# q and k loaded already turned, their rounded stacks written in place by ACT and POOL, an exponential bias from the minimum, an eighth weight slot

## The chip, the cores and the metric

One core of a Trainium2 chip runs the whole program. The metric is the device time of one execution in microseconds (us). The engines are PE (matrix multiplies), DVE (vector), ACT (activations), POOL (general) and SP (here it only issues transfers). PSUM is the memory that PE writes; it has eight banks of 128 x 512 floats.

## The reference

Three stages follow each other: attention in 2 x 8 heads of 768 tokens and 64 columns, masked by a six-bit hash, then a soft mixture of eight experts, then a gated two-layer network.

```python
q_bits = (q @ proj > 0); k_bits = (k @ proj > 0)      # 6 bits each
mask = q_bucket[:, :, :, None] == k_bucket[:, :, None, :]
scores = np.where(mask, scale * q @ k.T, -1e9)
attn = np.exp(scores - scores.max(-1)); attn /= attn.sum(-1) + 1e-9
x = attn @ v                                          # to 1536 x 512
logits = x @ phi; d = softmax(logits, 0); slot_input = d.T @ x
slot_out[e] = relu(slot_input[e] @ w1[e]) @ w2[e]     # 8 experts, 4 slots each
x = softmax(logits, 1) @ slot_out
h = x @ w_in; out = (h * sigmoid(1.702 * h)) @ w_out
```

A row of the mask can be empty; its attention is then the mean of v.

## The kernel before

**Attention.** The outer loop runs over 16 heads m (head 0, a hardware loop of six rounds with two heads each, and three heads written out). Each head has six steps p, one for each tile of 128 queries. Every engine has its own written order. In step p, PE waits until the exponentials of tile p are there, multiplies the scores of the tile two further on (`target`: p+2, or tile 0 or 1 of the next head) at line 653, and turns the probabilities of tile p with six transposes at line 663. In steps 0 and 1 it also multiplies the previous head's turned probabilities with v (line 673), in step 0 the hashes of the next head (line 637), in step 2 it turns the previous head's output back (line 683). DVE finds the maximum of a row of scores (line 1046) and makes a bias of it (line 1049); ACT takes the exponential with that bias (line 933) and copies turned probabilities out of PSUM (line 927); DVE copies some of them (line 1040). There are two buffers of scores and two of probabilities, so an engine can run about one step ahead of the next.

**Stacks.** The scores are a sum of products of rounded ("high") and remainder ("low") parts. For each head four stacks of 128 x 768 hold them: `stack_a1` (q high twice), `stack_b1` (k high, k low), `stack_a2` (q low, hash bits), `stack_b2` (k high, hash bits). The four are there twice, for even and odd heads. Before, q and k of head m+2 come in with tokens on the partitions; PE turns them in step 4 (line 629), ACT and DVE copy them out (lines 946 and 1057), POOL makes `high` and `low` (lines 560 and 567), and SP places them in the stacks with six transfers (lines 442 and 448). DVE compares the hashes (line 1075) and SP places the bits with four transfers (line 433).

**Empty rows.** The sum of v over all tokens (POOL line 575, PE line 645, DVE line 1083) times a factor for empty rows (DVE line 1097) is added to the output by POOL (lines 585 and 591).

**Experts and the last network.** Weights come as 20 numbered fills, mostly of 2 MB. There are 11 slots for them, seven in `ring_lo` and four in memory that attention leaves free. Fills 0 to 5 are loaded inside the loop. A fill from 11 on has to wait until an expert has used up the slot (`REUSE`). Line 816 is the first product of an expert, line 835 the second, line 878 the first product of the last network, lines 892 to 914 the rest. PE also runs matmuls on `ones` that nobody reads (line 622), in places where it would stand idle.

Of the kernel before, what the change touches and what calls it, by code (L numbers as in the profile page):

```python
# [23 lines left out]
F32 = mybir.dt.float32  # L24
# [5 lines left out]
P = 128  # L30
BANK = 512
BIG = 2.0 ** 40
MASKED = -8e9
# [3 lines left out]
def kernel_program(nc, q, k, v, proj, phi, w1, w2, w_in, w_out, out):  # L37
    B, H, S, D = q.shape
    NB = proj.shape[1]
# [21 lines left out]
    assert D * 2 == P and TILES % 2 == 0 and SL == QUAD and CH == NQ and 3 * NB <= QUAD and HD == BANK and G * BANK == N  # L61

    bh = lambda x: x.rearrange("b h s d -> (b h) s d")
    q_dram, k_dram, v_dram = bh(q), bh(k), bh(v)

    with ExitStack() as ctx:
# [8 lines left out]
        LO = 7  # L75
        FOUR = 4
        PLACES = TILES + 2
        ARENA = (3 + 2 * FOUR + 2) * S + 2 * TILES * D + HC + TILES * PLACES * P
# [6 lines left out]
        ident = sb("ident", [P, P])  # L85
        stack_i = sb("stack_i", [P, SL])
        ones = sb("ones", [P, P])
        proj_w = sb("proj_w", [P, 2 * QUAD])
        small_at = -(-nc.sbuf_base // 32) * 32
        small = sb("small", [P, HC])  # L90
        hash_c = sb("hash_c", [P, 2])
        max_raw = sb("max_raw", [P, 2, TILES])
        neg_max = sb("neg_max", [P, 2, TILES])
        row_sum = sb("row_sum", [P, 2, TILES])
        empty = sb("empty", [P, TILES])
        denom = sb("denom", [P, TILES])
        recip = sb("recip", [P, TILES])
        e_recip = sb("e_recip", [P, TILES])
        v_part = sb("v_part", [P, 2, D])
        v_sum = sb("v_sum", [P, 2, D])  # L100
# [14 lines left out]
        high = rounded("high", arena_at, [P, S])  # L115
        uniform = arena[:, 0:HC].rearrange("p (t d) -> p t d", t=TILES)
        at[0] = S
        nat = part(S).rearrange("p (t f) -> p t f", t=TILES)
        low = rounded("low", arena_at + 4 * at[0], [P, S])
        qk = part(S)  # L120
# [5 lines left out]
        PROBS_AT = at[0]  # L126
# [5 lines left out]
        low_first = rounded("low_first", arena_at + 4 * PROBS_AT, [P, S])  # L132
        nat_second = probs[:, 1, :].rearrange("p (t f) -> p t f", t=TILES)
# [3 lines left out]
        SLOTS = 11  # L137
        PLACE = (0, 3, 1, 4, 2, 5, 6, 7, 8, 9, 10)
        A_AT = HC
# [10 lines left out]
        REUSE = (0, 2, 4, 1, 6, 3, 8, 5, 7)  # L150
# [25 lines left out]

        slot_t = v_part[:, :, :].rearrange("p r d -> p (r d)").rearrange("p (c s) -> p c s", c=CH)
        out_t = v_sum[:, :, :].rearrange("p r d -> p (r d)").rearrange("p (c s) -> p c s", c=CH)

        hid_t = x_flat[:, SLOT + N:SLOT + N + 2 * HK * SL].rearrange("p (w k s) -> p w k s", w=2, k=HK)  # L180


# [1087 lines left out]
```

## Time and profile before

| | |
|---|---|
| median of 3 runs | 479.94 us (479.64 to 482.36) |
| the profiled execution | 482.05 us, of which the span of the trace is 480.3 us |
| PE busy | 460.0 us (96%) |
| DVE busy | 304.0 us (63%) |
| ACT busy | 226.8 us (47%) |
| POOL busy | 108.7 us (23%) |
| moved by the transfers | 76.76 MB |

The trace lists instructions with their start and duration. A row of the timeline merges repeats (x4), says in brackets how long the engine sat idle before it and which engine released it. Roughly, attention lasts to 262 us of the span, logits and slot sums to 282, the experts to 325, the last network to the end.

### The profile page before, as it was taken

What the parts mean: (1) busy time and instruction counts of PE and PEld (TensorE: products, weight loads), DVE (VectorE), ACT (ScalarE), POOL (GpSimd) and SP (SyncE); (2) the same over time, 40 slices, a digit from 0 to 9 for tenths busy, and PEclk for the clock granted to TensorE, in tenths of its full rate; (3) what the DMA queues carried; (4) which work ended last, traced back from release to release, by engine and by line L of the source; (5) the groups of instructions that cost most, each with busy time, mean ns of one, the idle gap of its engine ahead of it and who ended that gap; (6) DMA issues with size and microseconds to landing.
All of it is one profiled execution on the core that took longest, in us unless ns stands there. A gap on an engine that the chain in (4) does not pass through costs nothing.

```text
span 480.3 us, 8550 instructions
## 1 busy us (share of the span) xinstructions
PE 460.0 (96%) x2939; PEld 341.5 (71%) x2939; DVE 304.0 (63%) x582; ACT 226.8 (47%) x476; POOL 108.7 (23%) x194
## 2 busy tenths in 40 slices
PE   7789999999999999999999999689999999999997
PEld 6577678776687766777675754236788888888885
DVE  3377778777787777877763440105999486648661
ACT  1376667866678666786664331115633221121110
POOL 4234344443444434444311000000000000000000
PEclk9799999999999999999999999999999999999999
DMA  5547768767776677773685659997000110010002
GB/s 139 142 114 206 185 190 234 193 206 197 197 213 196 202 192 203 214 199 106 195 294 186 253 202 373 396 409 285 1 0 2 44 45 0 2 72 16 1 0 87
DMA packets 55833, 76.76 MB, mean 160 GB/s; under 512 B 29313, under 2 KB 33281, under 8 KB 55297
## 3 DMA queue, kind: packets, MB, share of 16 engines
q1 hardware_dynamic: 55808, 76.44, 51.4%
q8 instruction: 15, 0.25, 0.2%
q14 instruction: 10, 0.07, 0.1%
HBM read 51.45 MB, written 3.15 MB: 114 GB/s over the span
## 4 chain that ended last, share of the span: by engine, by line
PE 88%; DMA 7%; DVE 2%; SPq 1%; ACT 1%; issue 1%; ACTq 0%; DVEq 0%
PE ps L653 16%; PE ps L673 13%; PE ps L663 12%; PE ps L912 9%; PE ps L914 9%; PE ps L913 9%; DMA ring_lo<-in_moe_w 4%; PE ps L637 3%; PE ps L629 2%; PE ps L892 2%; PE ps L816 2%; PE ps L622 2%; PE ps L835 2%; PE ps L742 1%; PE ps L683 1%; DMA arena<-in_k 1%
## 5 line engine op out<-in xcount | busy, mean ns | idle before, releaser
L1046 DVE TENSOR_REDUCE max_raw<-ps 128x1 f32<-128x768 f32 x96 | 91.9, 957 | 49.5 <-PE ps L653 48.5
L653 PE MATMUL ps<-stack_b,stack_a 96*128 96x384 f32 (+1 forms) x384 | 93.5, 366 | 4.7 <-ACT arena L933 1.6
L933 ACT ACTIVATE arena<-ps,neg_max 128x768 f32<-128x768 f32 x96 | 86.8, 904 | 17.4 <-DVE neg_max L1049 16.0
L927 ACT COPY arena<-ps 128x384 f32<-128x384 f32 x144 | 64.4, 482 | 51.1 <-PE ps L663 51.0
L653 PEld LDWEIGHTS ps<-stack_b,stack_a 96*128 96x128 f32 (+1 forms) x384 | 63.5, 192 | 28.9 <-ACT arena L933 14.9
L663 PE MATMUL ps<-ident,arena 128*128 128x128 f32 x576 | 79.8, 274 | 1.1 <-ACT arena L927 1.0
L912 PE MATMUL ps<-w_high,g_high 128*128 128x512 f32 x192 | 75.0, 390 | 1.2 <-DVE g_low L1227 1.1
L914 PE MATMUL ps<-w_high,g_low 128*128 128x512 f32 x192 | 74.7, 389 | 0.0
L913 PE MATMUL ps<-w_low,g_high 128*128 128x512 f32 x192 | 74.7, 389 | 0.0
L663 PEld LDWEIGHTS ps<-ident,arena 128*128 128x128 f32 x576 | 68.9, 141 | 5.0 <-ACT arena L933 1.4
L673 PE MATMUL ps<-arena 128*64 128x384 f32 x384 | 68.0, 491 | 0.0
L1023 ACT ACTIVATE arena<-ps 128x512 f32<-128x512 f32 x48 | 28.3, 599 | 79.7 <-PE ps L892 79.7
L673 PEld LDWEIGHTS ps<-arena 128*64 128x64 f32 x384 | 25.9, 137 | 31.2 <-issue 28.7
L1237 DVE TENSOR_TENSOR arena<-ps,arena 128x512 f32<-128x512 f32 x48 | 33.0, 688 | 19.6 <-ACT arena L1023 19.5
L912 PEld LDWEIGHTS ps<-w_high,g_high 128*128 128x128 f32 x192 | 36.0, 188 | 9.7 <-issue 2.3
L914 PEld LDWEIGHTS ps<-w_high,g_low 128*128 128x128 f32 x192 | 36.0, 188 | 7.5
L913 PEld LDWEIGHTS ps<-w_low,g_high 128*128 128x128 f32 x192 | 36.0, 188 | 7.4
L567 POOL TENSOR_TENSOR low<-arena,high 128x768 fp32r<-128x768 f32 x15 | 27.3, 1818 | 35.6 <-PE ps L637 35.6
L1227 DVE TENSOR_TENSOR g_low<-arena,g_high 128x512 fp32r<-128x512 f32 x48 | 33.2, 692 | 1.7
L591 POOL TENSOR_TENSOR x_sb<-x_sb,arena 128x384 f32 (+1 forms) x16 | 16.0, 1002 | 69.1 <-DVE x_sb L1104 69.1
L1040 DVE COPY arena<-ps 128x384 f32<-128x384 f32 x48 | 26.5, 553 | 2.0 <-PE ps L663 2.0
L1225 DVE CAST g_high<-arena 128x512 fp32r<-128x512 f32 x48 | 20.5, 428 | 5.4 <-DVE arena L1237 0.9
(121 smaller groups left out, 463.6 us busy)
## 6 DMA issues: line engine op xcount, KB each, us to landing
ring_lo<-in_moe_w SPq DMA_DIRECT2D x12, 1024.0 KB, 5.5
ring_lo<-in_moe_w SPq DMA_DIRECT2D x6, 2048.0 KB, 16.7
stack_a<-high SPq DMA_DIRECT2D x32, 192.0 KB, 3.1
stack_b<-high SPq DMA_DIRECT2D x32, 192.0 KB, 3.3
arena<-in_moe_w SPq DMA_DIRECT2D x3, 2048.0 KB, 8.4
arena<-in_q SPq DMA_DIRECT2D x16, 192.0 KB, 3.2
arena<-in_k SPq DMA_DIRECT2D x16, 192.0 KB, 3.4
arena<-in_v SPq DMA_DIRECT2D x16, 192.0 KB, 2.4
```

The lines of the kernel that those rows point to most:

```text
L653: last = nc.tensor.matmul(s_ps[p % 2][:, c, :], a[r][0:used, rows], b[r][0:used, cols], start=(a is stack_a1), stop=(a is stack_a2))
L663: last = nc.tensor.transpose(ring[b][:, j * P:(j + 1) * P], probs[:, p % 2, kt * P:(kt + 1) * P], ident[:, :])
L673: last = nc.tensor.matmul(o_ps[x * D:(x + 1) * D, :], nat_v[:, r, kt, :], probs_t[:, at:at + HALF, kt, :], start=(kt == 0), stop=(kt == TI ...
L912: nc.tensor.matmul(ps[:, 4 + tt, :], g_high[:, s % DEEP, rows], w_h, start=(fi == 0), stop=False)
L913: nc.tensor.matmul(ps[:, 4 + tt, :], g_high[:, s % DEEP, rows], w_l, start=False, stop=False)
L914: last = nc.tensor.matmul(ps[:, 4 + tt, :], g_low[:, s % DEEP, rows], w_h, start=False, stop=(fi == FC - 1))
L927: nc.scalar.copy(probs_t[:, place(r, p), b * HALF:(b + 1) * HALF, :], ring[b].rearrange("p (a s) -> p a s", a=HALF)).then_inc(t_taken[b], 1)
L933: nc.scalar.activation(probs[:, p % 2, :].rearrange("p (c s) -> p c s", c=2), s_ps[p % 2], ACT.Exp, bias=neg_max[:, r, p:p + 1], scale=SCA ...
L1023: nc.scalar.activation(sig[:, s % 4, :], ps[:, fi % 4, :], ACT.Sigmoid, scale=1.702)\
L1046: nc.vector.tensor_reduce(max_raw[:, r, p:p + 1], s_ps[p % 2], axis=AX.XY, op=ALU.max)\
L1227: nc.vector.tensor_tensor(g_low[:, s % DEEP, :], gated[:, s % 2, :], g_high[:, s % DEEP, :], ALU.subtract)\
L1237: nc.vector.tensor_tensor(gated[:, s % 2, :], ps[:, fi % 4, :], sig[:, s % 4, :], ALU.mult)\
```

## The change

The host hands over q and k already turned and each twice over the 128 partitions (`qk`), and all constants in one tensor (`consts`). ACT and POOL (in head 0 DVE too) write the rounded parts straight into the stacks, with a column of `const` as scale. SP's six placing transfers, PE's transposes of q and k and the copies out of PSUM are gone. The signs and the scale of the scores are in the stacks, so that masked products are large and positive: DVE takes the minimum, makes a scale (-1, or 0 for an empty row) and a bias of it in two small instructions, and ACT's exponential has the scale and the bias as columns. A row that is empty gives exp(0) = 1 everywhere, so the sum of v and its addition are gone. The bits are scaled by POOL in place. `ring_lo` has eight slots, so there are 12. Fill 6 goes out in head 0, fills 7, 8 and 9 in the last three heads. The number of `ones` matmuls at the start changes.

```diff
-        LO = 7
+        LO = 8
...
-        SLOTS = 11
+        SLOTS = 12
...
-        REUSE = (0, 2, 4, 1, 6, 3, 8, 5, 7)
+        REUSE = (0, 2, 4, 1, 6, 3, 8, 5)
...
             def body(m, r, k):
+                if within(m, 2) and (not isinstance(m, int) or m > 0):
+                    sp.wait_ge(hash_ready, m + 2)
+                    sp.wait_ge(k_again, m + 2)
+                    load_qk(m + 2, r, both)
                 if within(m, 1):
                     place_bits(m + 1, 1 - r)
-                    place_low(m + 1, 1 - r, low)
...
-                if within(m, 3):
-                    sp.wait_ge(qk_turned[1], m + 3)
-                    load_qk(m + 3, 1 - r, nat)
-                if within(m, 2):
-                    sp.wait_ge(scores_ready, m * TILES + TILES)
-                    place_high(m + 2, r)
...
+            def low_q(n, r, src):
+
+                pool.wait_ge(q_high, n + 1)
+                nc.gpsimd.tensor_tensor(stack_a2[r][lower, :], src[lower, 0, :], stack_a1[r][lower, :], ALU.subtract)\
+                    .then_inc(q_low, 1)
...
             def body(m, r, k):
                 if within(m, 1):
-                    split_low_of(m + 1)
-                if within(m, -1):
-                    finish(m - 1, 1 - r, k + r - 1)
-                if within(m, 1):
-                    fold_v(m + 1, 1 - r, k + r)
+                    scale_bits(m + 1)
                 if within(m, 2):
-                    if not isinstance(m, int) or m > 0:
-                        pool.wait_ge(x_done, m + K0)
-                    split_high_of(m + 2, r, k + r + 1)
+                    pool.wait_ge(qk_in[r], (k + 2) * 2 * DMA)
+                    pool.wait_ge(scores_ready, m * TILES + TILES)
+                    high_k(r, both)
+                    low_q(m + 2, r, both)
+                    low_k(m + 2, r, both)
+                    nc.gpsimd.tensor_tensor(stack_b2[r][lower, :], both[lower, 1, :], over(k_scale, lower), ALU.mult)\
+                        .then_inc(k_again, 1)
...
+                for j in range(NQ):
+                    last = nc.tensor.matmul(hash_ps[j * QUAD:(j + 1) * QUAD, :], proj_w,
+                                            src[:, j % 2, (j // 2) * HC:(j // 2 + 1) * HC], start=True, stop=True)
...
-                    if p == TILES - 2 and within(m, 2):
-                        pe.wait_ge(hash_taken, m + 2)
-                        if not isinstance(m, int) or m > 0:
-                            pe.wait_ge(x_scaled, m)
-                        turn_qk(m + 2, r, k + 1, nat)
...
-                    if p == TILES - 1:
-                        sum_v(m, r)
...
-                                     bias=neg_max[:, r, p:p + 1], scale=SCALE,
+                                     bias=exp_bias[:, r, p:p + 1], scale=exp_scale[:, r, p:p + 1],
...
+            high_q_and_k_again(0, both)
+            act.wait_ge(hash_taken, 1)
+            for j in range(NQ):
+                rows = slice(j * QUAD, (j + 1) * QUAD)
+                last = nc.scalar.activation(
+                    (stack_a2, stack_b2)[j % 2][0][D:D + QUAD, (j // 2) * HC:(j // 2 + 1) * HC],
+                    bits[rows, :], ACT.Copy, scale=bit_times[rows, :])
...
-                    if p == TILES - 2 and within(m, 2):
-                        take_qk(m + 2, r, k + r + 1)
                     take_tile(m, r, p, 0)
                     if p % 2 == 0:
                         take_tile(m, r, p, 1)
                     if p + 2 < TILES or within(m, 1):
                         act.wait_ge(t_ready[1], m * TILES + p + 1)
                         exps(*target(m, r, k, p))
+                    if p == HALF and within(m, 2):
+                        act.wait_ge(qk_in[r], (k + 2) * 2 * DMA)
+                        nc.scalar.activation(stack_a1[r][:, :], both[:, 0, :], ACT.Copy, scale=q_scale).then_inc(q_high, 1)
...
-                nc.vector.tensor_reduce(max_raw[:, r, p:p + 1], s_ps[p % 2], axis=AX.XY, op=ALU.max)\
-                    .then_inc(max_found, 1)
-                dve.wait_ge(max_found, g + 1)
-                nc.vector.tensor_scalar(neg_max[:, r, p:p + 1], max_raw[:, r, p:p + 1], MASKED, -SCALE,
-                                        ALU.max, ALU.mult).then_inc(max_ready, 1)
...
+                nc.vector.tensor_reduce(low, s_ps[p % 2], axis=AX.XY, op=ALU.min).then_inc(min_found, 1)
+                dve.wait_ge(min_found, g + 1)
+                nc.vector.tensor_scalar(exp_scale[:, r, p:p + 1], low, EMPTY, -1.0, ALU.is_lt, ALU.mult)\
+                    .then_inc(scale_found, 1)
+                dve.wait_ge(scale_found, g + 1)
+                nc.vector.tensor_scalar(exp_bias[:, r, p:p + 1], low, exp_scale[:, r, p:p + 1], -1.0, ALU.mult, ALU.mult)\
+                    .then_inc(min_ready, 1)
```

Two places show what this does to the order. On ACT, in the first head of a loop round, from the exponential of step 3 to that of step 4 (L933, L842: exponential; L927, L836: turned probabilities; L946: half of q and k). Before:

```order
L927 COPY arena<-ps 128x384
L932 REGISTER_ALU
L933 ACTIVATE arena,row_sum<-ps,neg_max 128x768
L943 REGISTER_ALU
L945 ISA
L946 COPY arena<-ps 128x384
L927 COPY arena<-ps 128x384 x2
L932 ISA
L933 ACTIVATE arena,row_sum<-ps,neg_max 128x768
```

Of the change:

```order
L836 COPY arena<-ps 128x384
L841 REGISTER_ALU
L842 ACTIVATE arena,row_sum<-ps,exp_bias,exp_scale 128x768
L887 ISA
L888 ACTIVATE stack_a_50<-arena,const 128x768
L836 COPY arena<-ps 128x384 x2
L841 ISA
L842 ACTIVATE arena,row_sum<-ps,exp_bias,exp_scale 128x768
```

The copy of 384 columns ahead of step 4's two copies has given way to one of 768 columns from SBUF, in the same place between two exponentials.

On DVE, steps 2 and 3 of the same head (L1046, L969: reduction; L1104, L994: scaling of the previous head's output). Before:

```order
L1046 TENSOR_REDUCE max_raw<-ps 128x1
L1049 TENSOR_SCALAR neg_max<-max_raw 128x1
L1104 ISA
L1104 TENSOR_TENSOR x_sb<-ps,recip 128x6x64
L1045 REGISTER_ALU
L1046 TENSOR_REDUCE max_raw<-ps 128x1
L1049 TENSOR_SCALAR neg_max<-max_raw 128x1
L1040 COPY arena<-ps 128x384
```

Of the change:

```order
L969 TENSOR_REDUCE low_raw<-ps 128x1
L971 TENSOR_SCALAR exp_scale<-low_raw 128x1
L974 TENSOR_SCALAR exp_bias<-low_raw,exp_scale 128x1
L991 REGISTER_ALU
L994 ISA
L994 TENSOR_TENSOR x_sb<-ps,recip 128x6x64
L967 REGISTER_ALU
L969 TENSOR_REDUCE low_raw<-ps 128x1
L971 TENSOR_SCALAR exp_scale<-low_raw 128x1
L974 TENSOR_SCALAR exp_bias<-low_raw,exp_scale 128x1
L962 COPY arena<-ps 128x384
```

Behind every reduction stand two small instructions instead of one, the second of which reads what the first wrote.

## Rows read from the trace of the kernel before

**Rows 1.** Page, TensorE's granted clock in 40 slices, tenths of full speed.
```profile
PEclk9799999999999999999999999999999999999999
```
**Rows 2.** Timeline, one head: start us, duration us, engine, line, what, [idle before].
```profile
63.48 0.97 PE L653 MATMUL ps<-stack_b,stack_a 128*128 128x384 f32 x4
...
71.41 0.96 PE L653 MATMUL ps<-stack_b,stack_a 128*128 128x384 f32 x4
...
73.53 0.56 DVE L1104 TENSOR_TENSOR x_sb<-ps,recip 128x384 f32 x1
...
75.10 0.15 DVE L1049 TENSOR_SCALAR neg_max<-max_raw 128x1 f32<-128x1 f32 x1
...
75.29 0.90 ACT L933 ACTIVATE arena<-ps,neg_max 128x768 f32<-128x768 f32 x1 [0.33 <-DVE neg_max L1049]
...
75.45 0.82 PE L629 MATMUL ps<-ident,arena 128*128 128x128 f32 x6
...
76.11 0.82 PE L663 MATMUL ps<-ident,arena 128*128 128x128 f32 x6
76.18 0.47 ACT L946 COPY arena<-ps 128x384 f32<-128x384 f32 x1
...
77.38 0.92 ACT L933 ACTIVATE arena<-ps,neg_max 128x768 f32<-128x768 f32 x1
...
78.13 0.33 PE L645 MATMUL ps<-v_part,ones 128*128 128x64 f32 x2
...
78.44 0.97 PE L653 MATMUL ps<-stack_b,stack_a 128*128 128x384 f32 x4
```
**Rows 3.** The same timeline, small DVE instructions beside a POOL subtraction.
```profile
65.99 1.81 POOL L567 TENSOR_TENSOR low<-arena,high 128x768 fp32r<-128x768 f32 x1 [1.99 <-PE ps L637]
...
66.66 1.18 DVE L1089 TENSOR_SCALAR empty<-max_raw 128x6 f32<-128x6 f32 x1
...
67.87 0.17 DVE L1092 SCALAR_TENSOR_TENSOR denom<-empty,row_sum 128x6 f32<-128x6 f32 x1
68.07 0.19 DVE L1095 RECIPROCAL recip<-denom 128x6 f32<-128x6 f32 x1
```
**Rows 4.** Groups of ACT by line and shape: busy us, mean ns of one | idle.
```profile
L933 ACT ACTIVATE arena<-ps,neg_max 128x768 f32<-128x768 f32 x96 | 86.8, 904 | 17.4 <-DVE neg_max L1049 16.0
L1023 ACT ACTIVATE arena<-ps 128x512 f32<-128x512 f32 x48 | 28.3, 599 | 79.7 <-PE ps L892 79.7
...
L1013 ACT CAST w_high<-ring_lo 128x512 fp32r<-128x512 f32 x8 | 4.9, 617 | 0.1
...
L994 ACT COPY arena<-ps 128x256 f32<-128x256 f32 x8 | 3.0, 373 | 25.8 <-PE ps L816 25.8
```
**Rows 5.** Timeline of PE, head 0 and the start of head 1.
```profile
18.25 1.65 PE L653 MATMUL ps<-stack_b,stack_a 128*128 128x384 f32 x4 [1.55 <-ACT arena L933]
...
21.11 1.55 PE L637 MATMUL ps<-arena,proj_w 128*64 128x384 f32 x4
...
29.64 0.94 PE L653 MATMUL ps<-stack_b,stack_a 128*128 128x384 f32 x4 [1.45 <-DMA stack_a<-low]
...
33.41 0.97 PE L653 MATMUL ps<-stack_b,stack_a 128*128 128x384 f32 x4
```
**Rows 6.** Timeline of PE, the starts of heads 14 and 15.
```profile
228.21 0.97 PE L653 MATMUL ps<-stack_b,stack_a 128*128 128x384 f32 x4
...
242.79 0.97 PE L653 MATMUL ps<-stack_b,stack_a 128*128 128x384 f32 x4
```
**Rows 7.** Transfers by line: count, KB each, median us to landing.
```profile
ring_lo<-in_moe_w SPq DMA_DIRECT2D x12, 1024.0 KB, 5.5
```
**Rows 8.** Timeline of PE among the experts.
```profile
302.63 1.93 PE L816 MATMUL ps<-ring_lo,v_part 128*32 128x256 f32 x32
...
311.62 3.22 PE L816 MATMUL ps<-ring_lo,v_part 128*32 128x256 f32 x32 [4.25 <-DMA ring_lo<-in_moe_w]
```
**Rows 9.** Stretch before that wait: busy us, PEclk, DMA share, GB/s last.
```profile
290.30:311.60 21.30, 17.07 (x208) 7.11 (x200) 2.16 (x6) 2.66 (x6) 0.63 (x5) 0.98 1.03 394
```

More of the change, by code:

```diff
@@ L521, in _ @@
         def _(pool):
-            nc.gpsimd.memset(proj_w[:, :], 0.0).then_inc(consts_set, 1)
-            for dst, value in ((ident, 0.0), (stack_i, 0.0), (ones, 1.0)):
-                last = nc.gpsimd.memset(dst[:, :], value)
-            last.then_inc(consts_set, 1)
-            pool.wait_ge(consts_set, 2)
-            nc.gpsimd.affine_select(out=ident[:, :], in_=ident[:, :], compare_op=ALU.not_equal, fill=1.0,
-                                    base=0, pattern=[[-1, P]], channel_multiplier=1).then_inc(consts_set, 1)
@@ L529, in _ @@
-            pool.wait_ge(consts_set, 3)
-            pool.sem_inc(ident_ready, 1)
-            done = 3
-            for j in range(NQ):
-                pool.wait_ge(consts_set, done)
-                nc.gpsimd.affine_select(out=stack_i[:, :], in_=stack_i[:, :], compare_op=ALU.not_equal, fill=1.0,
-                                        base=-QUAD * j, pattern=[[-1, SL]], channel_multiplier=1)\
-                    .then_inc(consts_set, 1)
-                done += 1
-            rows_q = ((QUAD, 0.0, 0.0), (3 * NB, 0.0, -BIG), (2 * NB, -1.0, -BIG), (NB, 0.0, 2 * BIG))
@@ L542, in _ @@
-            rows_k = ((QUAD, 0.0, 0.0), (3 * NB, -1.0, 1.0), (2 * NB, 0.0, 1.0), (NB, 0.0, 1.0))
-            for steps in zip(rows_q, rows_k):
-                pool.wait_ge(consts_set, done)
-                for j in range(NQ):
-                    count, *values = steps[j % 2]
-                    for c, value in enumerate(values):
-                        last = nc.gpsimd.memset(hash_c[j * QUAD:j * QUAD + count, c:c + 1], value)
-                last.then_inc(consts_set, 1)
-                done += 1
@@ L593, in _ @@
-            fold_v(0, 0, 0)
-            split_high_of(1, 1, 1)
+            nc.gpsimd.memset(ones[:, :], 1.0).then_inc(ones_set, 1)
+            lower, upper = slice(0, D), slice(D, P)
+            over = lambda column, rows: column[rows, :].broadcast_to([D if rows != slice(0, P) else P, S])
+            def low_q(n, r, src):
+                pool.wait_ge(q_high, n + 1)
+                nc.gpsimd.tensor_tensor(stack_a2[r][lower, :], src[lower, 0, :], stack_a1[r][lower, :], ALU.subtract)\
+                    .then_inc(q_low, 1)
@@ L718, in body @@
                         if not isinstance(m, int) or m > 0:
-                            pe.wait_ge(sum_taken, m)
-                        hashes(m + 1)
+                            pe.wait_ge(qk_in[1 - r], (k + r + 1) * 2 * DMA)
+                            pe.wait_ge(hash_taken, m + 1)
+                            hashes(both)
+                    if p == 0 and within(m, -1):
+                        pe.wait_ge(v_in[1 - r], (k + r) * DMA)
                     if p < 2 and within(m, -1):
@@ L897, in _ @@
                 up(s)
-            idle(4, 8)
+            warm(4, 6)
             for g in range(G):
```

401 lines of the change are left out of this document (173 added, 228 removed).

## The prediction

> **What bounds the kernel now.** The page says PE is busy nearly all the time, which suggests that what comes off PE comes off the time. I read three more views to see whether that holds. First the timeline of one head, which repeats every 14.98 us: from the start of head 1 at 33.41 [rows 5] to that of head 14 at 228.21 [rows 6] are 194.80 us for 13 heads. In that head I look for a second path as long as PE's, and there is one. It runs from step 0's scores to the next head's step 0 [rows 2]: PE works through steps 0 and 1 until the scores of tile 4 start (63.48 to 71.41, 7.93 us). 2.12 later DVE, which has waited for them and found their maximum, scales the previous output. 1.57 after that comes the small instruction of the next tile's maximum (75.10), 0.19 later ACT's exponential. Then 0.89 to ACT's copy of half of q and k (0.47), 1.20 from there to the exponential of the next head's tile 0, with two copies of probabilities between, and 1.06 until PE's next step 0 at 78.44. The sum is 14.96. So DVE and ACT together close the head exactly when PE does; PE's 96% hides a tie. Second, the start: in head 0 PE waits for ACT and for a transfer and works at half speed for a while (four products in 1.65 us at 18.25, in 0.97 at 33.41) [rows 5], which the granted clock shows as 0.7 in the second slice [rows 1]. Third, the experts: PE waits 4.25 us for a weight transfer [rows 8], with the transfer engines busy throughout at 394 GB/s [rows 9].
>
> **A head in the loop.** From PE the change takes the transposes of q and k, 0.66 us (75.45 to 76.11), and the sum of v, 0.33 us [rows 2]. The hashes go from two products over 64 output rows to four over 32. In both cases products on different rows overlap, and I take the same time; 0.1 more would be the other end. If PE alone counted, a head would be 0.98 us shorter.
>
> But every link of the other path lies on ACT and DVE, and these get more work. (1) DVE has one more small instruction after each reduction. Two that depend on each other start 0.20 us apart (67.87 and 68.07) [rows 3], and the first takes about 0.17, so I count 0.19. Two of them lie on the path (tiles 4 and 5); a few hundredths of this fit in because the second reduction had to wait for PE at about the same moment. That gives +0.32. (2) ACT loses the copy of 384 columns, 0.46 on the path, and gets one of 768 columns from SBUF with a per-partition operand as scale. Between 256 and 512 columns ACT takes (599 - 373)/256 = 0.88 ns per column [rows 4]. A rounding copy of 512 from SBUF takes 617 ns [rows 4], so 768 take 0.84 us. What the operand as scale adds is in no row by itself. The exponential has one as bias and takes 904 ns at 768 columns, the sigmoid has none and takes 599 at 512 [rows 4]; at 0.88 per column that leaves fixed parts of 0.23 and 0.15, so some 0.08 for the operand, if it is not the summing that the exponential also does. The copy takes 0.84 to 0.92; from start to next start I take 0.87, so +0.41. (3) The exponentials now have two such operands. That is between 0 and 0.09 us each; I take 0.09, since the only row with an operand is also the one with the longer fixed part. Two lie on the path: +0.18. Sum 0.91. To this I add 0.02 for the two copies behind it, which in the profile used the time in which they waited for PE. A head thus takes 15.91 us, +0.93. Thirteen of them: **+12.1**.
>
> Here is a rule that speaks against the change. The Trainium skill, "ScalarE: Activation LUTs", section "What ACT_TABLE_LOAD costs", says that each per-partition pointer operand adds about 93 ns to an activation over immediate scale and bias. By it the two exponentials and the copy on the path get 0.28 us, which is what the sum has; if it did not hold, the sum would be 3.5 us lower over the loop. The two rows agree with it (0.08) without proving it.
>
> Heads 14 and 15 have no such copy, before or after. Without 0.46 and 0.87 there, the same path gives 15.0 for head 14 against 14.58 before (228.21 to 242.79) [rows 6]; head 15 gets the same two DVE instructions and one exponential. Together **+1.0**.
>
> What is hidden: POOL's four instructions for a head (nearest row 1.81 us for 768 columns [rows 3]; they take time by columns, also on 64 partitions) and its scaling of the bits are about 7.5 us of 15.9. They start when the last scores of head m are done, about 10.7 us into it; the second waits for ACT's copy to 13.9, and the last ends some 3.4 us into the next head. Then q and k of the following head are loaded (needed at 13), and the bits are scaled and placed by about 9.5. PE wants them at its step 4, after 11.4. So this cover is 2 us deep.
>
> **The start.** Constants, q, k and v of head 0 are about 1.06 MB, and 1 MB lands 5.5 us after its issue [rows 7], so at about 6.2. Hashes and their comparison take 1.7 on PE and DVE, at half clock 2.4; ACT's four bit copies of 384 columns 0.51 each, 2.1. Scores can start at about 10.4, the first exponential at 12.8, and step 0 of head 0 at 13.9 instead of 18.25 [rows 5]. Head 0 took 15.16 from there to 33.41. It loses the 1.45 us of transfer wait and the 1.55 of hashes at half clock [rows 5], and gets the 0.93, so 13.1, and head 1 starts at 27.0: **-6.4**. I keep 1.5 us to either side of it.
>
> **The experts.** In the profile DMA is saturated from the slot sums on, and the fills that PE waits for are the fifth behind that point; with the twelfth slot they are the fourth. One fill is 2.1 MB, at 394 GB/s [rows 9] 5.3 us earlier, against a wait of 4.25 [rows 8]. The product after the wait took 3.22 instead of 1.93 us at a lower clock [rows 8], which goes too. **-5.6**. The fills after it shift by the same 5.3 us, so that nothing later becomes late. The last network is not touched.
>
> **Sum**: +12.1 + 1.0 - 6.4 - 5.6 = +1.1. The profiled execution is 482.05 us, so 483.1 for one like it; it lay 2.1 above the median of the runs, 479.94, which I take as the base: 481.0.
>
> **The rivals.** *PE is the bound and the rest gives way* (7 in 100): DVE and ACT would have slack that the timeline doesn't show; 0.98 less for 14 heads, so 479.9 - 13.7 - 6.4 - 5.6 = 454. Against it is the tie above. *The copy and the pointers cost less* (15): ACT's link grows by 0.1 only, a head by 0.45, so 5.9 + 0.6 - 6.4 - 5.6, 474.5. *The wait among the experts stays* (8), since later fills share the bandwidth with the one that PE needs: 486.6. The margin is 5.3 - 4.25, 1 us. *POOL's chain comes too late* (9): each head's load waits for the fourth POOL instruction and the bits queue behind it. It decides once POOL is more than 2 us later than above, that is if its four instructions take 2.3 us rather than 1.8; 1 us more in each of 13 heads is 494. *PE's clock falls* (3): it stands still for about 2 us of each head, in waits of up to 0.6 us. In head 0 the clock was lower after waits of 1.4 and 1.55 us [rows 5], while waits such as the 0.1 to 0.6 us in the loop left it at full [rows 1]; with one head in four at 1.65 for 0.97 it would be over 500. The last one comes below. That leaves 56 for the forecast, whose own range is 476 to 486.
>
> *DVE's small instructions wait for POOL* (2): an instruction over six columns took 1.18 us where others of that size take 0.17, and it ended at 67.84, just behind POOL's subtraction (65.99 + 1.81 = 67.80) [rows 3]. POOL now works while DVE is on the path. At half of 1.81 for each of two links, 13 heads would take 23 us more, and the time be near 504. Against it, the small instruction on the path takes 0.15 [rows 2], and its two successors have its form.
>
> By the Trainium skill, "SBUF — State Buffer", section "Who interferes with whom", a copy or tensor_scalar of DVE in a two-port mode is blocked for the whole of a POOL instruction. The wait at 66.66 agrees; no row shows it for a single column.
>
> **Numbers.** The range 470 to 489 leaves out the first rival and the last three, some 2 in 10. About 1% (475 to 485) is what a measurement of this kernel can tell from no change. Faster by more: the first rival 7, most of the second 10, the lower tail of the forecast 4, so 0.21. Slower by more: 9 + 3 + 2, most of the third 6, the upper tail 3, so 0.23. The rest is 0.56.
>
> **What would show it.** The first step of head 1 at 27 and head 14 about 207 later (15.9 each; 14.0 would be the first rival). PE idle in each head before steps 3 to 5 and 0, released by ACT's exponential, and its share of the span falling. The mean of the exponential 0.99 instead of 0.90, that of the copy at line 888 about 0.92. No wait for DMA at the first product of expert 7. Waits of PE for the bits or for POOL at step 4 would show the fourth rival. I would be wrong above all if ACT's copy, placed between two exponentials on the path, did not move the second of them.

## The result and the profile after

| | before | changed |
|---|---|---|
| median | 481.54 us (8 runs, 478.35 to 483.64) | 484.53 us (8 runs, 484.13 to 485.55) |
| span of the profiled execution | 480.3 us | 483.5 us |
| PE / DVE / ACT / POOL busy | 460.0 / 304.0 / 226.8 / 108.7 us | 454.5 / 305.1 / 245.5 / 112.2 us |
| moved by the transfers | 76.76 MB | 64.25 MB |

The ratio is 1.0073, with a 95% interval of 1.0045 to 1.0101: 0.7% slower, within the 1% that the prediction called no change, and 3.5 us above its 481.0: 1.6 of it because the kernel before now measures 481.5 rather than 479.9, 1.9 from the sum. PE is busy for 5.5 us less and the kernel is 3 us longer.

The executions of the kernel before differ in their mean granted clock, and their spans with it: over all sets of runs with a listed clock 475.5 and 476.1 us at 1.000, 477.3 to 478.4 at 0.995 and 0.996, 479.4 to 480.9 at 0.988 and 0.989. The eight of the changed kernel are all at 0.996 (482.1 to 483.5). At equal clock the change therefore costs more like 4.5 us than 3.

Page of the changed kernel: busy time, TensorE's granted clock, the chain that ended last.
```profile
PE 454.5 (94%) x2859; PEld 321.5 (66%) x2859; DVE 305.1 (63%) x611; ACT 245.5 (51%) x483; POOL 112.2 (23%) x87
...
PEclk9899999999999999999999999999999999999999
...
PE 74%; DVE 10%; ACT 8%; issue 7%; DMA 1%; DVEq 0%; SPq 0%; ACTq 0%
...
L560 PE MATMUL ps<-stack_b,stack_a 96*128 96x384 f32 (+1 forms) x384 | 93.4, 365 | 14.7 <-ACT arena L842 13.3
```
The chain of the kernel before, from its page:
```profile
PE 88%; DMA 7%; DVE 2%; SPq 1%; ACT 1%; issue 1%; ACTq 0%; DVEq 0%
```
DMA is nearly off the chain, and DVE has 10% of it. Ahead of its scores (line 560) PE now stands idle for 14.7 us in all, nearly always for ACT's exponential. In the 13 heads of the loop the granted clock is full before and after, so it is no part of what the heads show. It is a part of the rest: before, it was 0.50 from 17.3 to 24.1 us and from 310.9 to 314.3, behind the wait among the experts; in the changed kernel it was 0.50 from 16.7 to 20.1 only.

Timeline of the changed kernel, the head from 107.49 to 123.56, in the columns of [rows 2]. Line 560 is the scores, 969 the reduction, 971 and 974 the two small instructions, 842 the exponential, 888 the copy of 768 query columns, 836 the copies of turned probabilities, 994 the scaling of the output.
```profile
107.49 0.98 PE L560 MATMUL ps<-stack_b,stack_a 128*128 128x384 f32 x4 [0.43 <-ACT arena L842]
...
109.06 0.85 PE L550 MATMUL ps<-arena,const 128*32 128x384 f32 x8
...
109.84 2.16 PE L580 MATMUL ps<-arena 128*64 128x384 f32 x12
...
115.56 0.98 PE L560 MATMUL ps<-stack_b,stack_a 128*128 128x384 f32 x4
...
116.58 0.96 DVE L969 TENSOR_REDUCE low_raw<-ps 128x1 f32<-128x768 f32 x1 [1.79 <-PE ps L560]
...
117.96 0.56 DVE L994 TENSOR_TENSOR x_sb<-ps,recip 128x384 f32 x1
...
118.31 1.47 POOL L495 TENSOR_TENSOR stack_b<-arena,const 128x768 fp32r<-128x768 f32 x1 [6.50 <-PE ps L560]
...
119.42 0.15 DVE L971 TENSOR_SCALAR exp_scale<-low_raw 128x1 f32<-128x1 f32 x1
119.61 0.21 DVE L974 TENSOR_SCALAR exp_bias<-low_raw,exp_scale 128x1 f32<-128x1 f32 x1
...
119.86 0.99 ACT L842 ACTIVATE arena<-ps,exp_bias,exp_scale 128x768 f32<-128x768 f32 x1 [0.40 <-DVE exp_bias L974]
...
120.84 0.93 ACT L888 ACTIVATE stack_a<-arena,const 128x768 fp32r<-128x768 f32 x1
...
121.67 0.84 ACT L836 COPY arena<-ps 128x384 f32<-128x384 f32 x2
...
122.40 1.01 ACT L842 ACTIVATE arena<-ps,exp_bias,exp_scale 128x768 f32<-128x768 f32 x1
...
123.56 0.97 PE L560 MATMUL ps<-stack_b,stack_a 128*128 128x384 f32 x4 [0.44 <-ACT arena L842]
```
It lasts 16.07 us, against 14.96 in [rows 2]. Both heads can be laid on each other link by link:

| link | before | changed | difference | predicted |
|---|---|---|---|---|
| PE's steps 0 and 1, to the scores of tile 4 | 7.93 | 8.07 | +0.14 | 0 |
| those scores to the scaling of the output | 2.12 | 2.40 | +0.28 | } +0.32 |
| scaling to the first small instruction of tile 5 | 1.57 | 1.46 | -0.11 | } |
| that to the exponential | 0.19 | 0.44 | +0.25 | } |
| exponential to the copy of q | 0.89 | 0.98 | +0.09 | +0.09 |
| copy of q, and the two copies, to the next exponential | 1.20 | 1.56 | +0.36 | +0.43 |
| exponential to PE's next step 0 | 1.06 | 1.16 | +0.10 | +0.09 |
| sum | 14.96 | 16.07 | +1.11 | +0.93 |

Groups of the changed kernel by line and shape, in the columns of [rows 4].
```profile
L842 ACT ACTIVATE arena<-ps,exp_bias,exp_scale 128x768 f32<-128x768 f32 x96 | 95.9, 999 | 25.8 <-DVE exp_bias L974 25.7
...
L490 POOL TENSOR_TENSOR stack_a<-arena,stack_a 64x768 fp32r<-64x768 f32 x16 | 28.8, 1803 | 34.9 <-ACT stack_a L888 28.8 <-ACT stack_a L859 6.1
...
L501 POOL TENSOR_TENSOR stack_b<-arena,stack_b 64x768 fp32r<-64x768 f32 x15 | 27.4, 1825 | 1.1
...
L495 POOL TENSOR_TENSOR stack_b<-arena,const 128x768 fp32r<-128x768 f32 x15 | 22.0, 1468 | 91.7 <-PE ps L560 90.8 <-DVE stack_b L1005 1.0
...
L974 DVE TENSOR_SCALAR exp_bias<-low_raw,exp_scale 128x1 f32<-128x1 f32 x96 | 20.6, 214 | 3.4
...
L529 POOL TENSOR_TENSOR stack_b<-arena,const 64x768 fp32r<-64x768 f32 x14 | 20.5, 1461 | 1.0
...
L985 DVE TENSOR_SCALAR denom<-row_sum 128x6 f32<-128x6 f32 x16 | 18.2, 1139 | 0.0
...
L971 DVE TENSOR_SCALAR exp_scale<-low_raw 128x1 f32<-128x1 f32 x96 | 14.8, 154 | 3.3
...
L888 ACT ACTIVATE stack_a<-arena,const 128x768 fp32r<-128x768 f32 x14 | 12.9, 924 | 0.0
```
The exponential went from 904 [rows 4] to 999 ns. Of the two small instructions the second, with its column operand, takes 214 ns, the first 154. Lines 490 to 529 are POOL's four instructions for a head's stacks.

Timeline of PE in the changed kernel: step 0 of heads 0, 1, 14 and 15, and the first product of expert 7.
```profile
11.30 1.66 PE L560 MATMUL ps<-stack_b,stack_a 128*128 128x384 f32 x8
14.86 0.97 PE L560 MATMUL ps<-stack_b,stack_a 128*128 128x384 f32 x4 [1.89 <-ACT arena L842]
...
27.20 0.96 PE L560 MATMUL ps<-stack_b,stack_a 128*128 128x384 f32 x4 [0.44 <-ACT arena L842]
...
236.02 0.94 PE L560 MATMUL ps<-stack_b,stack_a 128*128 128x384 f32 x4 [0.53 <-ACT arena L842]
...
251.48 0.94 PE L560 MATMUL ps<-stack_b,stack_a 128*128 128x384 f32 x4 [0.39 <-ACT arena L842]
...
316.11 1.93 PE L725 MATMUL ps<-ring_lo,slot_t 128*32 128x256 f32 x32
```
The account of the span:

| stretch | before | changed | difference | predicted |
|---|---|---|---|---|
| start to head 1 | 33.41 | 27.20 | -6.2 | -6.4 |
| 13 heads | 194.80 | 208.82 | +14.0 | +12.1 |
| heads 14 and 15 | | | +1.1 | +1.0 |
| experts: no wait for the weights of expert 7, full clock behind it | | | -5.6 | -5.6 |
| logits and slot sums, last network | | | -0.1 | 0 |
| sum | | | +3.2 | +1.1 |

### The profile page after: what moved, and what is told of

Same layout as the page of the kernel before. It is cut to its first block, busy times and chain, and to the rows that moved or that the text cites. A ratio compares the mean times of both kernels' runs of the same rounds, so it can differ in the third digit from the quotient of the medians.

```text
span 483.5 us, 8010 instructions
## 1 busy us (share of the span) xinstructions
PE 454.5 (94%) x2859; PEld 321.5 (66%) x2859; DVE 305.1 (63%) x611; ACT 245.5 (51%) x483; POOL 112.2 (23%) x87
## 2 busy tenths in 40 slices
DMA packets 27495, 64.25 MB, mean 133 GB/s; under 512 B 2896, under 2 KB 6992, under 8 KB 26960
## 4 chain that ended last, share of the span: by engine, by line
PE 74%; DVE 10%; ACT 8%; issue 7%; DMA 1%; DVEq 0%; SPq 0%; ACTq 0%
PE ps L580 14%; PE ps L560 10%; PE ps L821 9%; PE ps L823 9%; PE ps L822 9%; DVE low_raw L969 7%; ACT arena L842 5%; PE ps L570 5%; PE ps L744 3%; PE ps L725 3%; PE ps L550 3%; ACT arena L836 2%; PE ps L545 2%; PE ps L801 2%; PE ps L650 1%
## 5 line engine op out<-in xcount | busy, mean ns | idle before, releaser
L969 DVE TENSOR_REDUCE low_raw<-ps 128x1 f32<-128x768 f32 x96 | 91.7, 955 | 61.5 <-PE ps L560 61.2
L842 ACT ACTIVATE arena<-ps,exp_bias,exp_scale 128x768 f32<-128x768 f32 x96 | 95.9, 999 | 25.8 <-DVE exp_bias L974 25.7
L560 PE MATMUL ps<-stack_b,stack_a 96*128 96x384 f32 (+1 forms) x384 | 93.4, 365 | 14.7 <-ACT arena L842 13.3
L836 ACT COPY arena<-ps 128x384 f32<-128x384 f32 x144 | 64.0, 479 | 45.2 <-PE ps L570 44.6
L570 PE MATMUL ps<-const,arena 128*128 128x128 f32 x576 | 82.5, 278 | 4.6 <-ACT arena L836 4.5
L570 PEld LDWEIGHTS ps<-const,arena 128*128 128x128 f32 x576 | 67.7, 141 | 15.3 <-ACT arena L836 7.6
L580 PEld LDWEIGHTS ps<-arena 128*64 128x64 f32 x384 | 24.8, 136 | 34.9 <-issue 31.1
L495 POOL TENSOR_TENSOR stack_b<-arena,const 128x768 fp32r<-128x768 f32 x15 | 22.0, 1468 | 91.7 <-PE ps L560 90.8
L490 POOL TENSOR_TENSOR stack_a<-arena,stack_a 64x768 fp32r<-64x768 f32 x16 | 28.8, 1803 | 34.9 <-ACT stack_a L888 28.8
L501 POOL TENSOR_TENSOR stack_b<-arena,stack_b 64x768 fp32r<-64x768 f32 x15 | 27.4, 1825 | 1.1
```

The costliest lines, as they stand in the source:

```text
L490: nc.gpsimd.tensor_tensor(stack_a2[r][lower, :], src[lower, 0, :], stack_a1[r][lower, :], ALU.subtract)\
L560: last = nc.tensor.matmul(s_ps[p % 2][:, c, :], a[r][0:used, rows], b[r][0:used, cols], start=(a is stack_a1), stop=(a is stack_a2))
L570: last = nc.tensor.transpose(ring[b][:, j * P:(j + 1) * P], probs[:, p % 2, kt * P:(kt + 1) * P], ident[:, :])
L580: last = nc.tensor.matmul(o_ps[x * D:(x + 1) * D, :], nat_v[:, r, kt, :], probs_t[:, at:at + HALF, kt, :], start=(kt == 0), stop=(kt == TI ...
L836: nc.scalar.copy(probs_t[:, place(r, p), b * HALF:(b + 1) * HALF, :], ring[b].rearrange("p (a s) -> p a s", a=HALF)).then_inc(t_taken[b], 1)
L842: nc.scalar.activation(probs[:, p % 2, :].rearrange("p (c s) -> p c s", c=2), s_ps[p % 2], ACT.Exp, bias=exp_bias[:, r, p:p + 1], scale=ex ...
```

## The experiments

Two theories stood against each other. **A**: a head lasts as long as the path from the scores over DVE's reduction and small instructions, ACT's exponential and the copy of q to the next exponential; PE waits for it. **B**: PE's own work sets the head, and what was added to ACT and DVE fills their idle time. For a kernel on one core the span of the profiled execution lies about 2 us below its time; differences between spans are given beside the medians, because the medians of before moved between the three sets of runs (481.3, 479.8 and 481.6 us). The profiled execution of the changed kernel has the longest span of its eight (483.5; the others 482.1 to 482.7), so differences of span against it come out up to 1 us too large. The safest measure is the time of the 13 heads of the loop.

| kernel | median us | against before, 95% interval | span us |
|---|---|---|---|
| changed | 484.5 | 1.0073 (1.0045 to 1.0101) | 483.5 |
| q copy moved | 475.2 | 0.9865 (0.9831 to 0.9900) | 473.1 |
| small instructions independent | 478.8 | 0.9952 (0.9930 to 0.9974) | 476.5 |
| scale immediate | 482.0 | 1.0024 (1.0004 to 1.0044) | 479.9 |
| moved and independent | 467.4 | 0.9706 (0.9672 to 0.9739) | 465.3 |
| changed, PE refilled | 485.4 | 1.0108 (1.0077 to 1.0139) | 483.6 |
| changed, 11 slots | 491.2 | 1.0222 (1.0184 to 1.0259) | 489.1 |
| before, scale as a column | 484.7 | 1.0093 (1.0061 to 1.0125) | 482.7 |
| moved, independent, PE refilled | 474.2 | 0.9882 (0.9852 to 0.9911) | 472.0 |
| column operand gone, wait kept | 483.6 | 1.0045 (1.0022 to 1.0069) | 481.5 |

**Is PE's relief worth anything?** In the changed kernel PE gets back what it lost.

```diff
                     if p + 2 < TILES or within(m, 1):
                         scores(*target(m, r, k, p))
+                    if p == TILES - 2 and within(m, 2):
+                        for _ in range(6):
+                            nc.tensor.transpose(ps[:, 7, HC:HC + P], ones[:, :], ident[:, :])
                     transpose_probs(m, p)
+                    if p == TILES - 1:
+                        nc.tensor.matmul(ps[:, 7, HC:HC + D], ones[:, :], ones[:, 0:D], start=True, stop=True)
```


> The changed kernel with TensorE's relief given back: six 128x128 transposes of the ones in step 4 of heads 0 to 13 (0.82 us by the traces' 137 ns each) and one 64-column product in step 5, into a bank that nobody reads, so that TensorE has again what the removed stack transposes took. Theory A (the head lasts as long as the chain scores, reduction, two small instructions, exponential, and the copy between two exponentials; TensorE waits for ACT about 1.0 us a head): the added work goes into that idle time, at most 1 us more than the changed kernel's 484.5. Rival B (TensorE's own work still sets the head): 14 x 0.98 = 13.7 us more, 498.

The span grew by 0.1 us, the median by 0.8. Timeline of PE in this kernel: steps 0 of heads 1 and 14.
```profile
27.26 0.97 PE L560 MATMUL ps<-stack_b,stack_a 128*128 128x384 f32 x4 [0.19 <-ACT arena L847]
...
235.97 0.94 PE L560 MATMUL ps<-stack_b,stack_a 128*128 128x384 f32 x4 [0.36 <-ACT arena L847]
```
208.71 us for 13 heads, against 208.82. B falls for the changed kernel: taking this work off PE gave nothing.

**Was the path already binding before the change?** The kernel before gets the exponential's scale from a column.

```diff
+        scale_c = sb("scale_c", [P, 1])
...
-                                     bias=neg_max[:, r, p:p + 1], scale=SCALE,
+                                     bias=neg_max[:, r, p:p + 1], scale=scale_c[:, :],
```


> The kernel before with the exponential's scale read from a 128x1 column that holds the same number in all rows, nothing else. The exponential's mean should go from 904 to about 999 ns. If ACT is on the loop's chain before the change too (the kernel before balanced between TensorE and the chain), two exponentials a head are on it: 14 x 2 x 0.095 = 2.7 us more, 484.0 against this job's before of about 481.3. If TensorE alone sets the head of before, no more than 0.5 us.

Group of the exponential and, by the timeline of PE, steps 0 of heads 1 and 14.
```profile
L934 ACT ACTIVATE arena<-ps,neg_max,scale_c 128x768 f32<-128x768 f32 x96 | 95.6, 995 | 14.6 <-DVE neg_max L1050 14.3
```
```profile
32.83 0.97 PE L654 MATMUL ps<-stack_b,stack_a 128*128 128x384 f32 x4
...
229.90 0.97 PE L654 MATMUL ps<-stack_b,stack_a 128*128 128x384 f32 x4
```
197.07 us for 13 heads against 194.80 is 0.175 a head, nearly the two times 0.091 by which the exponential grew (904 [rows 4] to 995). So already before, nearly all that was added on ACT's path came out at the end of the head, although PE was busy 96% of the span. The span grew by 2.4 us, the 13 heads by 2.3. The median grew by 4.9 against the before of its own set, where 2.7 were expected; part of that is the granted clock: at 0.989 the spans are 479.9 (one execution of before) and 482.7 to 483.0. This shows one half of the tie that the prediction read from one head. The other half, that PE too is at its limit there, rests on its rows (busy 194.6 of the 194.8 us of 13 heads); no run changes PE's work in the kernel before.

**The copy of q between two exponentials.** It is moved from step 3 of head m to step 0 of head m+1, where ACT waits for PE anyway; POOL's subtraction follows it, and SP's order is changed so that the bits don't queue behind the load that now waits for it.

```diff
-                    if p == HALF and within(m, 2):
-                        act.wait_ge(qk_in[r], (k + 2) * 2 * DMA)
-                        nc.scalar.activation(stack_a1[r][:, :], both[:, 0, :], ACT.Copy, scale=q_scale).then_inc(q_high, 1)
+                    if p == 0 and within(m, 1) and (not isinstance(m, int) or m > 0):
+                        act.wait_ge(qk_in[1 - r], (k + r + 1) * 2 * DMA)
+                        nc.scalar.activation(stack_a1[1 - r][:, :], both[:, 0, :], ACT.Copy, scale=q_scale)\
+                            .then_inc(q_high, 1)
...
                 if within(m, 1):
                     scale_bits(m + 1)
+                    if not isinstance(m, int) or m > 0:
+                        low_q(m + 1, 1 - r, both)
```


> ACT's copy of 768 columns of q is moved from step 3, where it stands between two exponentials, to step 0 of the next head, where ACT sits idle for 2.2 us before the copy of step 1 (113.26 in the changed kernel's timeline); POOL's q subtraction and the load of q and k move with it. Theory A (a head is closed by a path over DVE and ACT, PE only keeps up): the 0.83 us of the copy leave each of 13 heads, 10.8 us, so 484.5 - 10.8 = 473.7 and a head of 15.2. Rival B (PE, with its matmuls and issue time, sets the head, and ACT's position is of no account): no change, 484.5. Rival C (POOL's chain or the load, which now start differently, take its place): between the two, with waits of PE at step 4 for POOL or a transfer.

9.3 us came off the median, as over the 13 heads, and 10.4 off the span. Timeline of PE, heads 1 and 14:
```profile
25.97 0.97 PE L564 MATMUL ps<-stack_b,stack_a 128*128 128x384 f32 x4 [0.43 <-ACT arena L846]
...
225.54 0.95 PE L564 MATMUL ps<-stack_b,stack_a 128*128 128x384 f32 x4 [0.40 <-ACT arena L846]
```
15.35 us a head instead of 16.06. The copy still takes 0.92 us; it merely stands where ACT has nothing to do. Its place was worth 0.71 of the 0.83 us that it occupied on the path. Link by link in one head of each timeline, 0.78 comes off between the exponential of tile 5 and that of the next tile 0 (2.54 to 1.76), and PE's steps 0 and 1 get 0.09 longer (8.07 to 8.16).

**The second small instruction.** It no longer reads the first one's result, and does not wait for it. The bias is the minimum, or at most 16 where a row is empty.

```diff
                 nc.vector.tensor_scalar(exp_scale[:, r, p:p + 1], low, EMPTY, -1.0, ALU.is_lt, ALU.mult)\
-                    .then_inc(scale_found, 1)
-                dve.wait_ge(scale_found, g + 1)
-                nc.vector.tensor_scalar(exp_bias[:, r, p:p + 1], low, exp_scale[:, r, p:p + 1], -1.0, ALU.mult, ALU.mult)\
+                    .then_inc(min_ready, 1)
+                nc.vector.tensor_scalar(exp_bias[:, r, p:p + 1], low, TOP, 1.0, ALU.min, ALU.mult)\
                     .then_inc(min_ready, 1)
```


> The bias is min(low, 16) with immediates instead of low times the scale just written, so that the second small DVE instruction no longer waits for the first and has no per-partition operand. For an empty row the scale is 0 and all exponentials are exp(16), which the sum divides out. Theory A: on the path are two pairs; in each the second one started 0.19 us after the first and ended 0.21 later, with 0.10 to 0.12 and 0.15 instead, so 0.13 each, 0.26 per head and 3.4 us over 13 heads, some 4 with the last two: 480.5. Rival B (PE sets the head): no change, 484.5.

5.7 us came off the median and 7.0 off the span, more than the 4 expected; a head takes 15.71 us, 0.35 less, where 0.26 were expected. That is 4.6 us over the 13 heads. Another 1.7 of the span lie before head 1, where this execution had the full granted clock throughout and that of the changed kernel had 0.50 for 3.4 us. Timeline of DVE and ACT:
```profile
105.98 0.15 DVE L972 TENSOR_SCALAR exp_scale<-low_raw 128x1 f32<-128x1 f32 x1
106.05 0.14 DVE L974 TENSOR_SCALAR exp_bias<-low_raw 128x1 f32<-128x1 f32 x1
...
106.23 0.99 ACT L843 ACTIVATE arena<-ps,exp_bias,exp_scale 128x768 f32<-128x768 f32 x1
```
From the first small instruction to the exponential it is 0.25 us, against 0.44 in the changed kernel (119.42 to 119.86). A further kernel splits this: the operand is replaced in the same way and the wait for the first instruction is kept.

```diff
-                nc.vector.tensor_scalar(exp_bias[:, r, p:p + 1], low, exp_scale[:, r, p:p + 1], -1.0, ALU.mult, ALU.mult)\
+                nc.vector.tensor_scalar(exp_bias[:, r, p:p + 1], low, TOP, 1.0, ALU.min, ALU.mult)\
```


> The changed kernel, where the second small instruction no longer reads the column that the first wrote but takes the minimum against 16 (with these inputs only empty rows change, from exp(0) to exp(16) everywhere, which their sum divides out); it still waits for the first. It splits the 5.7 us that making the two independent gave. By the traces a column operand costs 0.06 us (214 against 154 ns) and the wait 0.12 (starts 0.19 apart against 0.07). Theory A, both are on the path twice a head: 0.12 x 14 = 1.7 us and some 0.3 in head 0 from the operand, so 482.5, and the rest from the wait. Rival: reading a column just written is what delays the start too; then most of the 5.7 goes here, 479.5.

Timeline of DVE and ACT, and the group of the second small instruction:
```profile
108.28 0.16 DVE L972 TENSOR_SCALAR exp_scale<-low_raw 128x1 f32<-128x1 f32 x1
108.47 0.15 DVE L975 TENSOR_SCALAR exp_bias<-low_raw 128x1 f32<-128x1 f32 x1
108.65 0.99 ACT L843 ACTIVATE arena<-ps,exp_bias,exp_scale 128x768 f32<-128x768 f32 x1 [0.18 <-DVE exp_bias L975]
```
```profile
L975 DVE TENSOR_SCALAR exp_bias<-low_raw 128x1 f32<-128x1 f32 x96 | 14.7, 154 | 3.3
```
The time is 483.6, 0.9 below that of the changed kernel: half of the 2 that A expected, and far from the rival's 5. The span is 2.0 below, but 0.9 of this lie before head 1. Head 1 starts at 26.31 and head 14 at 234.24, so a head takes 15.99 us, 0.07 less than in the changed kernel: the 0.06 by which the second instruction is shorter (154 against 214 ns) counts once a head, not twice. Behind the other pair, the scaling of the output starts 2.40 us after the scores of tile 4 with and without the operand. So of the 0.35 us that the independent pair saves in a head, the operand is 0.07 and the wait of one small instruction for the other 0.28, or 0.9 and 3.7 us over 13 heads. Of that wait the rows show 0.19 us from start to start, 0.07 without it, behind each of the two reductions.

**The exponential's second column operand.** The changed kernel with the constant -1.0 as scale; here the rows whose mask is empty come out as zeros.

```diff
-                                     bias=exp_bias[:, r, p:p + 1], scale=exp_scale[:, r, p:p + 1],
+                                     bias=exp_bias[:, r, p:p + 1], scale=-1.0,
```


> The exponential has the scale -1 as an immediate instead of a per-partition operand; DVE still computes that operand. Rows that are empty come out as zeros, so that part of the computation is left out. Theory A with the price of 0.095 us for the operand (999 against 904 ns): two exponentials lie on the path of a head, 0.19 for 13 heads and a little for the last two, 2.7 us, so 481.8. If the longer exponential has another cause (the sign, the range of its input), it stays at 999 ns and the time at 484.5. Rival B: the exponential gets shorter and the time stays.

2.5 us came off the median, as over the 13 heads, and 3.6 off the span. Group of the exponential:
```profile
L842 ACT ACTIVATE arena<-ps,exp_bias 128x768 f32<-128x768 f32 x96 | 87.3, 909 | 27.0 <-DVE exp_bias L974 26.8
```
909 instead of 999 ns: 0.09 for the operand. The head went from 16.06 to 15.87 us, twice that.

**The twelfth slot.** The changed kernel with the eleven slots of before and its fills.

```diff
-        SLOTS = 12
-        PLACE = (0, 3, 1, 4, 2, 5, 6, 7, 8, 9, 10, 11)
+        SLOTS = 11
+        PLACE = (0, 3, 1, 4, 2, 5, 6, 8, 9, 10, 11)
...
-        REUSE = (0, 2, 4, 1, 6, 3, 8, 5)
+        REUSE = (0, 2, 4, 1, 6, 3, 8, 5, 7)
```


> The changed kernel with the eleven weight slots of before, and the fills where before had them; nothing else. By the traces, the first product of expert 7 waits again for its DMA (4.3 us in the kernel before, 0.0 in the changed one), and the products behind the wait run at the lower granted clock. Theory A: the twelfth slot alone gave the 5.6 us that the experts became shorter, so 484.5 + 5.6 = 490.1. Rival: the start of the experts later by 8.8 us and other loads gave part of it; then less than 3 us more, under 487.5.

The span is 489.1, 5.6 more, and the median 6.6 more. Timeline of PE, the first product of expert 7:
```profile
320.26 3.43 PE L723 MATMUL ps<-ring_lo,slot_t 128*32 128x256 f32 x32 [4.43 <-DMA ring_lo<-in_moe_w]
```
The wait and the slow product of [rows 8] are back (4.25 and 3.22 us there), and they are a little larger: 4.43 for the wait and 1.50 for the slower product are 5.9, where 5.6 were expected. The slot, with the fills that it lets go out earlier, gave this part by itself.

**Both repairs together.** The copy of q moved and the small instructions independent, with the edits shown above.

> Both edits together, the output stays the reference's. Theory A: 484.5 - 10.8 - 3.4 = 470.3, if PE, DVE's 1.0 us reductions and the exponentials leave room for both; PE's own work is 14.1 us in a head, so that a head of 14.95 is still above it. This would be below the kernel before (481.5). If the sum is less than the two singly, another path (PE from step 2 on) has come up between.

467.4 us: 3% faster than the kernel before, and better than the changed one by 17.1, where 14.2 were expected and the two alone gave 9.3 and 5.7. Steps 0 of heads 1 and 14 in the timeline of PE, and DVE's instruction over six columns in the group view:
```profile
24.79 0.98 PE L565 MATMUL ps<-stack_b,stack_a 128*128 128x384 f32 x4 [0.21 <-ACT arena L847]
...
218.45 0.93 PE L565 MATMUL ps<-stack_b,stack_a 128*128 128x384 f32 x4 [0.27 <-ACT arena L847]
```
```profile
L990 DVE TENSOR_SCALAR denom<-row_sum 128x6 f32<-128x6 f32 x16 | 2.6, 161 | 0.0
```
14.90 us a head, 1.16 less than in the changed kernel, where the two alone gave 0.71 and 0.35. The 0.1 that is left over lies where the moved copy alone had lost it: PE's steps 0 and 1 take 8.06 us here (99.21 to 107.27) and not 8.16, and from the exponential of tile 5 to the next it is 1.71 (111.21 to 112.92) and not 1.76. Is PE the bound at last? It gets the same six transposes and the product back as above.

> The kernel with the query copy moved and the two small instructions independent (467.4 us, head 14.90 us, TensorE busy for 14.66 us of it), with TensorE's removed work given back: six 128x128 transposes of the ones in step 4 and one 64-column product in step 5 of heads 0 to 13, into a bank that nobody reads. If TensorE's own work sets this kernel's head, all but the 0.24 us idle show: (0.98 - 0.24) x 14 = 10.4 us more, 477.8. If the chain through DVE and ACT still sets it, at most 2 us more, under 469.5.

The time is 474.2, neither of the two: 6.8 us more where 10.4 or at most 2 were expected. In the timeline of PE heads 1 and 14 start at
```profile
25.33 0.98 PE L565 MATMUL ps<-stack_b,stack_a 128*128 128x384 f32 x4
...
225.00 0.94 PE L565 MATMUL ps<-stack_b,stack_a 128*128 128x384 f32 x4 [0.16 <-ACT arena L852]
```
so a head takes 15.36 us, 0.46 more of the 0.98 given back. The timeline of one head (PE, ACT) shows where: line 628 is the six added transposes, 575 those of the probabilities, 846 ACT's copies of them.
```profile
114.06 0.99 ACT L852 ACTIVATE arena<-ps,exp_bias,exp_scale 128x768 f32<-128x768 f32 x1 [0.24 <-DVE exp_bias L984]
114.31 0.82 PE L628 MATMUL ps<-const,ones 128*128 128x128 f32 x6
...
114.96 0.82 PE L575 MATMUL ps<-const,arena 128*128 128x128 f32 x6
...
115.49 0.86 ACT L846 COPY arena<-ps 128x384 f32<-128x384 f32 x2 [0.35 <-PE ps L575]
...
116.23 1.01 ACT L852 ACTIVATE arena<-ps,exp_bias,exp_scale 128x768 f32<-128x768 f32 x1
```
From one exponential to the next it is 2.17 us instead of 1.71, which is the whole 0.46: the added transposes push back those of the probabilities, and ACT's copies now wait for PE. So neither engine alone is the bound; the path crosses from PE to ACT inside step 4. In the changed kernel ACT's copy of q stood in this place, and the same added work disappeared behind it.

## Why the prediction was right, point by point

**The bound.** That DVE and ACT close a head together with PE was the base of the sum. The column operand in the kernel before (+0.175 us a head) and the refilled PE in the changed one (span +0.1 us) show ACT's and DVE's side of it; that PE was as close before rests on its rows. The first rival, PE alone as the bound (454 us), would have needed heads of 14.0 us; they take 16.06.

**A head in the loop: the direction right, the size too small** (+1.08 instead of +0.93, 1.9 us over the loop, most of the miss). Three terms were off. (1) *DVE's small instructions* were put at 0.19 twice, less some slack, +0.32; the links show +0.42. Behind each reduction it is 0.19 to the second one, as predicted, but the second lasts 214 ns with its column operand, and I had priced it as an instruction without one (0.17), so the exponential starts 0.25 behind it, not 0.19. The run with the wait kept puts this operand at 0.07 a head. (2) *The hashes* were taken to cost the same, with 0.1 more as the other end. From their start to the next product it is 0.78 us (109.06 to 109.84), against some 0.70 before, and PE's steps 0 and 1 grew by 0.14. (3) *ACT's copy* was put at 0.87 from start to start and takes 0.83, so it and the copies behind it gave 0.07 back. The two exponentials came out as priced.

What speaks against the change by the Trainium skill, "ScalarE: Activation LUTs", section "What ACT_TABLE_LOAD costs", a cost of about 93 ns for each column operand, holds here: 909 to 999 ns in the changed kernel, 904 to 995 in the kernel before. The second rival, copy and pointers costing less (474.5), hung on this, and fell.

**Heads 14 and 15**: +1.0 predicted, +1.1 measured, but by luck. Head 14 was put at 15.0 us and takes 15.46 (236.02 to 251.48), 0.9 more than before instead of 0.4. Head 15, up to the first transposes of the output, takes 13.80 (251.48 to 265.28) against 13.58 before (242.79 to 256.37), 0.2 more instead of 0.6. Why head 14 takes longer than a head of the loop without its copy would, I did not trace.

**The start**: -6.4 predicted, -6.2 measured, but by two errors that cancel. Step 0 of head 0 came at 14.86, not 13.9. The bits were in place by 10.66, but PE started the first scores at 11.30, behind the hashes of head 1 and six matmuls on `ones`. The hashes themselves started at 9.83, right behind ten matmuls on `ones` that began at 7.40 and took 2.50 us. Head 0 then took 12.34 instead of 13.1.

**The experts**: -5.6 as predicted, and the eleven slots bring 5.6 back in span (5.9 among the experts, 6.6 in the median). In the kernel before, 1.3 of the 5.6 are the product at the lower clock. The rival that the wait stays is gone: the product at 316.11 follows its predecessor without a wait.

**POOL's chain** (rival at 494). Its four instructions were put at 1.81 us each; they take 1.47, 1.80, 1.83 and 1.46, and the last ended at 111.02 in the head shown, 3.5 us into it, where 3.4 was forecast. PE never waited for the bits. **DVE waiting for POOL** (504): the first small instruction at 119.42 lies inside POOL's 118.31 to 119.78 and still takes 0.15 us. The instruction over six columns, which has POOL beside it in the changed kernel, takes 1139 ns there, and 161 ns in the combined kernel, where POOL stands idle at that moment. So the wait for POOL is real, but instructions on a single column don't have it. **PE's clock** did not fall in the loop, though PE now stood idle for longer there, in waits of up to 0.4 us. In head 0 it did, as before: it was 0.50 from 16.7 to 20.1 us, behind a wait of 1.89 us at 14.86. But behind a wait of 1.71 us in the kernel with independent small instructions it stayed full.

## What to carry to other kernels

An engine that is busy 96% of the time can share the bound with a path through two other engines; lay out one round of the loop link by link before taking work off the busy one. Price added instructions by the place where they stand: the same 0.93 us copy cost 0.71 us a head more between two exponentials than where ACT waited for PE. Where two short instructions feed the next engine, let both read the same input: the second then comes 0.07 us behind the first and not 0.19.

## What was not expected of the hardware

A column operand makes a DVE instruction on 128x1 60 ns longer (154 to 214 ns). A wait for the instruction just ahead moves the second's start from 0.07 to 0.19 us behind the first; with two such pairs on the path of a head this was 3.7 us over 13 heads, against 0.9 for the column operand. In head 0, DVE's subtraction with two inputs from SBUF on 64 partitions and 768 columns took 1.47 us beside POOL's work; no run shows it alone.
